# Eleven key transposes moved from TensorE to VectorE, and three kinds of steps reordered, in a fused gated-attention and two-MLP kernel

## The reference

```
f = 1 / (1 + exp(-f_logit))
for t in range(S):                                    # S = 768, B x H = 4 x 8, D = 48
    state = f[:, :, t, :, None] * state + einsum('bhd,bhe->bhde', k[:, :, t], v[:, :, t])
    y[:, :, t] = einsum('bhd,bhde->bhe', q[:, :, t], state)
x = y, heads joined                                   # 3072 x 384
h = x @ w_in                                          # 384 -> 2048
g = where(h >= 1, h, where(h <= -1, 0, (h + 1)**2 / 4))
x = g @ w_out                                         # 2048 -> 384
h = x @ w_in2
P = a0 + a1*h + a2*h**2 + a3*h**3;  Q = 1 + |b0|*|h| + |b1|*h**2
out = (P / (Q + 1e-6)) @ w_out2
```

## Time and profile before

| | us |
|---|---|
| median of 3 timed executions | 914.7 (914.59, 914.70, 915.46) |
| the profiled execution, its own time | 913.45 |
| its span (first to last instruction) | 911.7 |
| TensorE busy | 885.8 (97% of the span) |
| VectorE busy | 665.3 (73%) |
| ScalarE busy | 631.9 (69%) |
| GpSimd busy | 271.0 (30%) |

### The profile page before, as it was taken

How to read it: one execution, slowest core, us unless ns; L and a number is a source line. 1 busy time by engine, 2 the same in 40 slices (tenths; PEclk the granted TensorE clock), 3 DMA queues, 4 the chain that set the end, 5 groups by cost and what they waited for, 6 DMA issues and landing times.

```text
span 911.7 us, 13158 instructions
## 1 busy us (share of the span) xinstructions
PE 885.8 (97%) x4786; PEld 732.0 (80%) x4786; DVE 665.3 (73%) x816; ACT 631.9 (69%) x822; POOL 271.0 (30%) x200
## 2 busy tenths in 40 slices
PE   4898999999999999999999999999999999999997
PEld 3787878888888888888888887888888888888886
DVE  8866666566555666565344799999899889989885
ACT  6766665655556555655567888888788888887873
POOL 3454400000100000000055385635344254343331
PEclk9999999999999999999999999999999999999999
DMA  8752122112111311200234121001001001000001
GB/s 216 192 167 59 37 68 72 36 35 87 36 36 36 98 51 35 79 26 1 84 91 137 44 63 36 1 35 35 0 35 35 12 22 35 30 5 0 35 0 38
DMA packets 26743, 48.70 MB, mean 53 GB/s; under 512 B 4544, under 2 KB 7616, under 8 KB 26688
## 3 DMA queue, kind: packets, MB, share of 16 engines
q1 hardware_dynamic: 26688, 47.99, 17.6%
HBM read 36.18 MB, written 9.44 MB: 50 GB/s over the span
## 4 chain that ended last, share of the span: by engine, by line
PE 81%; DVE 8%; ACT 4%; issue 4%; SPq 1%; DMA 1%; POOL 1%; POOLq 0%; DVEq 0%; ACTq 0%
PE acc L1233 19%; PE acc L1184 19%; PE h_pair L1167 17%; PE at_pair L1206 10%; PE h_pair L1206 10%; PE at_pair L1107 2%; PE at_pair L1126 2%; PE at_pair L1121 2%; DVE growth L869 1%; DVE g L940 1%; SPq L352 1%; DVE x_lo L933 1%; ACT t L664 1%; ACT t L661 1%; DMA q_in<-qC 1%
## 5 line engine op out<-in xcount | busy, mean ns | idle before, releaser
L559 POOL TENSOR_TENSOR g_lo<-g,g_hi 128x1024 fp32r<-128x1024 f32 x46 | 111.1, 2415 | 212.5 <-DVE t L984 212.5
L940 DVE SCALAR_TENSOR_TENSOR g<-h_pair,t 128x512 f32<-128x512 f32 x96 | 66.3, 691 | 137.0 <-ACT t L664 136.9
L661 ACT ACTIVATE t<-h_pair,half 128x512 f32<-128x512 f32 x96 | 66.0, 688 | 96.2 <-PE h_pair L1167 94.9
L1167 PE MATMUL h_pair<-x_hi,w_hi 128*128 128x512 f32 x288 | 113.0, 392 | 2.5 <-DVE x_lo L933 1.9
L522 POOL TENSOR_TENSOR k_s<-k_in,growth 128x512 f32<-128x512 f32 x22 | 28.9, 1315 | 286.0 <-DVE growth L869 268.9
L1233 PE MATMUL acc<-g_hi,w_hi 128*128 128x512 f32 x288 | 112.1, 389 | 0.3 <-POOL g_lo L559 0.3
L1167 PE MATMUL h_pair<-x_hi,w_lo 128*128 128x512 f32 x288 | 112.2, 390 | 0.0
L1167 PE MATMUL h_pair<-x_lo,w_hi 128*128 128x512 f32 x288 | 112.1, 389 | 0.0
L1233 PE MATMUL acc<-g_lo,w_hi 128*128 128x512 f32 x288 | 112.0, 389 | 0.0
L1233 PE MATMUL acc<-g_hi,w_lo 128*128 128x512 f32 x288 | 112.0, 389 | 0.0
L671 ACT CAST g_hi<-g 128x512 fp32r<-128x512 f32 x88 | 54.6, 620 | 81.5 <-DVE g L940 81.5
(11 more groups left out here) (171 smaller groups left out, 2045.7 us busy)
## 6 DMA issues: line engine op xcount, KB each, us to landing
w_raw<-w SPq DMA_DIRECT2D x32, 384.0 KB, 3.8
f_in<-fC SPq DMA_DIRECT2D x48, 96.0 KB, 2.9
k_in<-kC SPq DMA_DIRECT2D x48, 96.0 KB, 2.4
q_in<-qC SPq DMA_DIRECT2D x48, 96.0 KB, 2.3
mlp_out<-o_sb SPq DMA_DIRECT2D x18, 256.0 KB, 3.2
x_raw<-mlp_out SPq DMA_DIRECT2D x6, 768.0 KB, 4.5
outT<-o_sb SPq DMA_DIRECT2D x18, 256.0 KB, 2.0
v_in<-vC SPq DMA_DIRECT2D x22, 192.0 KB, 2.5
```

Source lines behind the costliest of these rows:

```text
L559: nc.gpsimd.tensor_tensor(g2_lo[r][:, :, :], g2[r][:, :, :], g2_hi[r][:, :, :].bitcast(F32), ALU.subtract).then_inc(lo2_ready, 1)
L661: nc.scalar.activation(t1[n % 2][:, :], h1[n % 2], ACT.Relu, scale=0.5, bias=half[:, :]).then_inc(relu1_ready, 1)
L940: nc.vector.scalar_tensor_tensor(out=g1[n % 2][:, :], in0=h1[n % 2], scalar=1.0, in1=t1[n % 2][:, :], op0=ALU.max, op1=ALU.min).then_inc(g ...
L1167: mm = nc.tensor.matmul(h1[n % 2], w[:, at:at + P], x[:, kt, cols], start=(kt == 0 and j == 0), stop=(kt == KT - 1 and j == 2))
```

## The change

For items 9 to 19 the keys are transposed by VectorE. TensorE's `transposes` and ScalarE's `copy_keys` do nothing for these items; in their place `turn_keys` issues 16 transposes of 32x32 blocks, each on 32 partitions x 128 elements (one quarter of the rows, one quarter of the columns of all four batches), from the scaled keys straight into `k_nat`. They are issued in five portions: 4 at stage 2 and 2 + 4 at stage 3 of the window before, 2 + 4 at stage 1 of the item's own. Items 0 to 8 keep the old path. `deltas` of such an item waits for the sixteen operations and for `states` of the item before; GpSimd's `scale_keys` waits for the sixteen of the item whose buffer it takes.

Two more moves hold for all windows: VectorE's `newton(i+1)` now stands between `spline_join` and `spline_lo` of stage 2, and at stages 1 to 3 ScalarE's `split_w1` stands between `spline_in` and `spline_hi` instead of at the step's end (at stage 0 its place stays).

```diff
+FIRST_TURNED = 2 * GROUPS + 1
+        def turned(i):
+            return FIRST_TURNED <= i < ITEMS - GROUPS
...
                 if before >= 0:
                     pool.wait_ge(scores_ready, before + 1)
-                    pool.wait_ge(kt_ready, min(before + 1, ITEMS - GROUPS))
+                    if before >= FIRST_TURNED:
+                        pool.wait_ge(turned_keys, 16 * (min(before + 1, ITEMS - GROUPS) - FIRST_TURNED))
+                    else:
+                        pool.wait_ge(kt_ready, before + 1)
...
             def copy_keys(i):
-                if i >= ITEMS - GROUPS:
+                if i >= ITEMS - GROUPS or turned(i):
                     return
...
                 if stage == 0:
                     copy_keys(i)
+                elif n <= PIECES - HEAD_PIECES:
+                    split_w1(n + HEAD_PIECES - 1)
                 if n < N1:
                     spline_hi(n)
+                if stage == 0 and n <= PIECES - HEAD_PIECES:
+                    split_w1(n + HEAD_PIECES - 1)
                 if stage == 1:
                     invert(i + 1)
...
-                if n <= PIECES - HEAD_PIECES:
-                    split_w1(n + HEAD_PIECES - 1)
...
+            def turn_keys(i, first, last):
+                if i >= ITEMS or not turned(i):
+                    return
+                dve.wait_ge(k_ready, i + 1)
+                dve.wait_ge(delta_ready, i - 1)
+                for k in range(first, last):
+                    q, j = k // (CK // SQ), k % (CK // SQ)
+                    src = k_scaled(i)[q * SQ:(q + 1) * SQ, :].rearrange("p (b t) -> p b t", b=BATCH)
+                    dst = k_natural(i)[j * SQ:(j + 1) * SQ, :].rearrange("p (b t) -> p b t", b=BATCH)
+                    nc.vector.transpose(dst[:, :, q * SQ:(q + 1) * SQ], src[:, :, j * SQ:(j + 1) * SQ]).then_inc(turned_keys, 1)
...
                 spline_join(n)
                 if stage == 0:
                     mask(i)
+                if stage == 1:
+                    turn_keys(i, 10, 12)
+                if stage == 2:
+                    newton(i + 1)
+                if stage == 3:
+                    turn_keys(i + 1, 4, 6)
                 spline_lo(n)
...
                 if stage == 2:
                     states(i)
                     if i % GROUPS == LAST:
                         rest_y(i)
-                    newton(i + 1)
                     scale_queries(i + 1)
+                    turn_keys(i + 1, 0, 4)
+                if stage == 1:
+                    turn_keys(i, 12, 16)
+                if stage == 3:
+                    turn_keys(i + 1, 6, 10)
...
             def transposes(i):
-                if i >= ITEMS - GROUPS:
+                if i >= ITEMS - GROUPS or turned(i):
                     return
...
             def deltas(i):
                 if i >= ITEMS - GROUPS:
                     return
-                pe.wait_ge(knat_ready, i + 1)
+                if turned(i):
+                    pe.wait_ge(turned_keys, 16 * (i + 1 - FIRST_TURNED))
+                    pe.wait_ge(delta_done, 2 * i)
+                else:
+                    pe.wait_ge(knat_ready, i + 1)
```

More of the change, by code:

```diff
@@ L14 @@
 HS = 64
+SQ = 32
 PAIRS = BATCH * HEADS // 2
@@ L226, in build @@
         knat_ready = sem("knat_ready")
+        turned_keys = sem("turned_keys")
         delta_ready = sem("delta_ready")
```

## The result

The changed kernel takes **902.74 us** (median of 4 executions, 902.63 to 902.77), the kernel before in the same session 915.08 (4 executions, 914.59 to 916.2): a ratio of 0.9867, 95% interval 0.9851 to 0.9882. The forecast was 904.5 with a range from 903.0 to 910.0. The profiled execution of before took 913.45 us (span 911.7), that of the change 902.77 (span 901.0): between the two traces lie 10.7 us, 0.2 of them ahead of step 0, where nothing was changed, so the change gave 10.5; the sum had 10.2. Between the medians lie 12.3.

A forecast was written before the change was run, and what follows sets the result against it. TensorE, busy all 20.59 us of a regular window, bounds the kernel, but waits for `rest_y` in early windows. -4.8 + 0.3 - 5.7 = -10.2 us takes the median from 914.7 to 904.5 us, range 903.0 to 910.0.

The forecast's parts named there:

- the sum: Whole kernel: transposes -4.8, second wait before `deltas` +0.3, early windows -5.7, together -10.2 us.
- Term 1: Items 9 to 19: transposes leave TensorE, 0.44 us an item, -4.8 us in all.
- Term 2: VectorE takes sixteen transposes a window at 0.30 us each, 4.8 us (3.1 to 6.4), reaching 17.2 us busy.
- +0.3 us: At `deltas` of eleven items: two waits in a row could expose a weight load, 0 to 1.1 us, taken as 0.3.
- Term 3: Steps 5 to 14: moved casts and `newton` shorten the ScalarE-VectorE loop, removing TensorE's waits for `rest_y`, -5.7 us (-6.3 to -4.6).
- relief from GpSimd: Steps 6 and 10: GpSimd works earlier, so `spline_lo` and `scale_queries` come free, 1.0 us a step, 2.1 us.
- first rival: Early windows: `rest_y` waits stay in part, their gain shrinks to -3 to 0, 907.2 to 910.2 us; chance 0.20.
- The second: Windows of items 9 to 19: VectorE becomes the bound at 0.73 us a transpose, 947 us; chance 0.06.
- The third: `deltas` in eleven windows: late by stage, not in sum, +1 to +4 us, 906 to 908.5; chance 0.06.
- its ends: Whole kernel: extremes of the forecast gain, -11.1 and -8.3 us, or 903.6 to 906.4 us.

The follow-up runs named there:

- doubled kernel: Every VectorE transpose issued twice, the second into a spare tile nothing reads, against the changed kernel: 910.16 us, 7.4 us more.

## Why the prediction was right, and where it was wrong

- **Term 1**, the transposes on TensorE: forecast 0.44 us an item and 4.8 in all, measured 0.46 and 5.04. The 0.44 are there to the hundredth between `spline_first` and the scores; the other 0.02 follow behind the scores.
- **Term 2**, VectorE: forecast 0.30 us for a transpose, 0.19 to 0.40 as bounds; measured 0.33 from one to the next (302 ns each). The choice by the pairs that begin at different partitions was the right one: with the destination unchanged it would have been 0.24, as the doubled kernel shows. Window load 17 us as forecast; the sixteenth transpose 0.97 us ahead of `deltas`, forecast 1.1.
- The **+0.3 us** for the second wait before `deltas` did not come: 0.45 us from deltas to the next matmul before and after.
- **Term 3**, the early windows: forecast 5.7 us, measured 5.44. The casts alone gave 4.1 us for the 4.0 worked out, `newton` 1.2 to 1.5 for 1.4. The relief from GpSimd came in step 6 at its size but at other operations, which is luck. `spline_lo` was to come free and still took 1.22 us, since GpSimd's split lasts until 70.2:

```profile
66.66 0.68 DVE L897 TENSOR_TENSOR q_s<-growth,guess 128x512 f32<-128x512 f32 x1
67.38 1.11 DVE L899 SCALAR_TENSOR_TENSOR guess<-q_s,guess 128x512 f32<-128x512 f32 x1
68.42 1.22 DVE L972 TENSOR_TENSOR g_lo<-g,g_hi 128x512 fp32r<-128x512 f32 x1
```

`newton`, put at nothing, took 0.68 us in its first operation, where the trace before has 1.27 (at 69.63), and `scale_queries` 0.69 for 1.10: 1.1 us together with `spline_lo`, forecast 1.0. In step 14, where 0.75 us was to be lost, `spline_lo` did come free (0.69 for 1.35) and nothing was. `rest_y` of item 6 ended at 72.45, within the 72.2 to 73.2 given.
- The first rival (early waits stay in part) did not come about; with three more items on VectorE it does. The second was tested: its count of a full VectorE held, its price of a transpose did not. The third did not come about; the kernel with the late transposes shows its mechanism at a larger size.
- **The step that failed** is the sentence on the sum: the profiled execution "stood 1.25 us under the median, 914.7, which so goes to 904.5". It took the distance of a profiled execution from the median for a constant that carries over. It was not: the kernel before has executions near 913.3 and near 915.0, in the traces with a short and with a long stretch of low clock, and others up to 918.5. The trace was of the first kind, the three timed executions (914.6 to 915.5) nearer the second. The changed kernel has no such stretch at the early waits; its four executions lie within 0.14 us, its profiled one among them. So against the trace the change gives 10.5 us (forecast 10.2: 0.2 more from term 1, 0.3 not paid before `deltas`, 0.3 less from term 3), and against executions of the second kind 1.6 us more. Had the sum been put on the trace's own time alone, it would have read 903.2, and by its ends (11.1 us at most) the range would have begun below 902.7. That the time lies 0.26 us outside the range and not inside it is partly chance: it hung on which kind the few timed executions were. Term 3 also read the low clock behind item 6 wrongly, though its sum stands: the 1.3 us of slow matmuls cost this execution nothing in the end, because item 7's scores waited that much less; by this an execution without any fall would lose about the same 6.3 us, nearly all of it in waits (up to item 7's scores two traces show it, for what follows it is argued). What an execution can lose beyond it is the fall behind item 7, 1.6 us, and term 3 had no place for that.

By the exclusive lock that the Trainium skill describes in "SBUF — State Buffer", section "Who interferes with whom", VectorE's `newton` would have lost 2.4 us more over two steps. In the changed kernel, with GpSimd's split right over it (66.83 to 70.2 us), `newton`'s second operation took 1.11 us, as before: slowed, not blocked for a whole GpSimd operation, and here the measurement decides. In the kernel with only `newton` moved the same operation once took 1.67 us, beside a `scale_keys` of 1.74, which is close to what the lock would give (up to 1.7), so the rule is not refuted for every pair of operations.

The Trainium skill, "VectorE: DVE Perf Modes", section "Rules for kernel authors", gives a 128x128 transpose to TensorE whenever PSUM will do as its destination. That is not borne out here: 16 operations of 0.33 us on VectorE replaced 0.46 us on TensorE and the kernel became faster, because only one of these engines was full.

In the section "Two Vector instructions with no wait between them" of the same page the Trainium skill says that an instruction is held until every earlier one has finished when its input or its output starts in another quadrant (32 partitions) than the last one in the same memory. The doubled kernel agrees: within a pair the second starts 0.24 us after the first, which takes 0.30, and the next pair 0.29 after an operation of 0.26.

## What to carry to other kernels

Price work by the engine that is full where the work stands: here 5.3 us of VectorE's time for 0.46 us of TensorE's is a gain as long as VectorE has both the time (12.4 + 16 x cost under the window's length) and a place that ends before the first matmul that needs the result; one stage later the same work costs 20 us of waits. Where a trace shows the clock at its lower level behind a wait, count that loss as one that varies between executions, look whether a later wait takes it up, and ask of several executions which kind the trace is before a distance to the median is carried over. A change that takes the wait away takes away the falls behind that wait, and no more: the kernel with only the moves had 907.7 to 911.2 us, through falls at the start, and single executions of two kernels with transposes lay 1.4 us over their fellows, for a reason that was not traced.

## What was not expected of the hardware

The same wait of 2.3 us before item 6's scores was followed by a fall of the clock in one execution (0.90, 0.50, 0.75 in the three stretches of 2 us from 74) and by none in two others; there the fall came some 22 us later, behind item 7's wait, and took twice as much (3.4 us lost for 1.7). The first fall cost the kernel nothing, the second 1.6 us. A fall can also come at the start, at 20 to 30 us, in one execution of a kernel whose other trace has none, for 2.8 us of time.
